# Linear attention and two gated layers on one core: batch 0 begun by pairs of heads, its spread over all rows, a late cast moved

## What is computed

```
kv  = k^T v                         per batch and head, 64 x 64
out = q kv;  out = out / sqrt(mean(out^2) + 1e-6) * g_norm
x   = out, heads side by side       4608 x 512
x   = (sigmoid(x Wg) * (x Wv)) Wo   512 -> 1536 -> 512
h   = x W_in                        512 -> 2048
y   = piecewise(h) W_out            h if h >= 1, 0 if h <= -1, else (h+1)^2/4;  2048 -> 512
```

## Time and profile before

| | |
|---|---|
| median of three runs | 1667.77 us |
| the profiled execution | 1663.86 us, of which its span 1662.1 us |
| busy in the span | PE 1645.1, DVE 1217.0, ACT 885.3, POOL 195.8 us |
| granted TensorE clock, mean | 1.00 |
| DMA | 278.91 MB, mean 168 GB/s |

### The profile page before, as it was taken

How to read it: one execution, slowest core, us unless ns; L and a number is a source line. 1 busy time by engine, 2 the same in 40 slices (tenths; PEclk the granted TensorE clock), 3 DMA queues, 4 the chain that set the end, 5 groups by cost and what they waited for, 6 DMA issues and landing times. The chain is left out here.

```text
span 1662.1 us, 31802 instructions
## 1 busy us (share of the span) xinstructions
PE 1645.1 (99%) x12471; PEld 1616.1 (97%) x12471; DVE 1217.0 (73%) x1733; ACT 885.3 (53%) x1612; POOL 195.8 (12%) x258
## 2 busy tenths in 40 slices
PE   8999999999999999999999999999999999999999
PEld 5899999999999999999999999999999999999999
DVE  5666777777877675876778887777777687766664
ACT  5666666655555554544445655555555444444442
POOL 2300001014432220100002400000001200000000
PEclk9999999999999999999999999999999999999999
DMA  7534444334776778745344433333438964444450
GB/s 269 179 125 144 132 148 142 114 130 133 253 250 232 245 241 288 248 157 155 117 143 140 165 129 143 118 118 136 167 143 267 341 185 135 129 128 127 128 137 29
DMA packets 229317, 278.91 MB, mean 168 GB/s; under 512 B 33072, under 2 KB 172848, under 8 KB 229168
## 3 DMA queue, kind: packets, MB, share of 16 engines
q1 hardware_dynamic: 217104, 233.35, 42.4%
q0 software_dynamic: 12064, 43.52, 8.2%
HBM read 156.76 MB, written 120.06 MB: 167 GB/s over the span
## 5 line engine op out<-in xcount | busy, mean ns | idle before, releaser
L1584 PE MATMUL x<-t_hi,v_lo 128*128 128x288 f32 x1664 | 495.8, 298 | 2.4 <-DVE v_lo L1104 0.9
L1585 PE MATMUL x<-t_lo,v_hi 128*128 128x288 f32 x1664 | 491.2, 295 | 0.0
L1586 PE MATMUL x<-t_hi,v_hi 128*128 128x288 f32 x1664 | 489.8, 294 | 0.0
L1584 PEld LDWEIGHTS x<-t_hi,v_lo 128*128 128x128 f32 x1664 | 312.0, 188 | 7.2 <-issue 2.1
L1586 PEld LDWEIGHTS x<-t_hi,v_hi 128*128 128x128 f32 x1664 | 313.3, 188 | 0.0
L1585 PEld LDWEIGHTS x<-t_lo,v_hi 128*128 128x128 f32 x1664 | 312.5, 188 | 0.1
L1584 PE MATMUL y<-t_hi,v_lo 128*128 128x288 f32 x832 | 248.2, 298 | 0.5 <-DVE c L1107 0.2
L1585 PE MATMUL y<-t_lo,v_hi 128*128 128x288 f32 x832 | 245.6, 295 | 0.0
L1586 PE MATMUL y<-t_hi,v_hi 128*128 128x288 f32 x832 | 245.0, 294 | 0.0
L1584 PE MATMUL x<-v_hi,t_lo 128*128 128x256 f32 x576 | 163.3, 283 | 2.7 <-ACT o_kept L1070 2.5
L1585 PE MATMUL x<-v_lo,t_hi 128*128 128x256 f32 x576 | 163.1, 283 | 0.0
(11 more groups left out here) (187 smaller groups left out, 3505.7 us busy)
## 6 DMA issues: line engine op xcount, KB each, us to landing
g_scratch<-c_tile SPq DMA_DIRECT2D x128, 288.0 KB, 2.4
gq<-g_scratch SPq DMA_DIRECT2D x64, 512.0 KB, 6.2
h_scratch<-gate SPq DMA_DIRECT2D x192, 144.0 KB, 2.0
hq<-h_scratch SPq DMA_DIRECT2D x32, 864.0 KB, 5.1
stage<-w_in POOLq DMA_DIRECT2D x68, 256.0 KB, 3.8
kv_ring<-kv_in SPq DMA_DIRECT2D x30, 512.0 KB, 4.4
fold_hi<-v_hi SPq DMA_DIRECT2D x14, 896.0 KB, 5.4
fold_lo<-v_lo SPq DMA_DIRECT2D x14, 896.0 KB, 6.9
```

The source lines that it names most:

```text
L1584: nc.tensor.matmul(dst, s_lo, m_hi, start=start, stop=False, skip_group_check=True)
L1585: nc.tensor.matmul(dst, s_hi, m_lo, start=False, stop=False, skip_group_check=True)
L1586: return nc.tensor.matmul(dst, s_hi, m_hi, start=False, stop=stop, skip_group_check=True)
```

## The change

Batch 0's k and v are loaded by pairs of heads, in 512-byte pieces, into places of their own; g's load is third. TensorE makes pair 0's and 1's products and heads, their two mean squares, then pairs 2 and 3, and the spread of the first two pairs before the second two pairs' means. A first root, reciprocal and inverse split serves pairs 0 and 1, a second all four. The warming passes behind the first ten are gone. The spread uses all 128 rows (the inverse's other rows are zeroed). The low part of task 0's weights and the sums of task 1's go from VectorE to GpSimd. Batch 1's k-v chunks have five places and no waits; its products are made in step 0; its k-v copies are ScalarE's. In stage D, the cast of item 4 comes after the first `keep`. The diff, cut:

```diff
         def _(sp):
-            def load_first_kv(i):
-                rows = min(P, S - i * P)
-                sp.dma_start(first_chunk(i)[0:rows, :], kv_in[0, i * P:i * P + rows, :]).then_inc(first_kv_loaded[i], 16)
+            def load_first_kv(c):
+                for side in range(2):
+                    at = slice(DM * side + P * c, DM * side + P * (c + 1))
+                    sp.dma_start(first_kv[:, 0:KVC - 1, at],
+                                 kv_in[0, 0:N, at].rearrange("(i p) d -> p i d", p=P)).then_inc(first_kv_loaded[c], 16)
...
-            for i in range(KVC):
-                load_first_kv(i)
-            for c in range(K):
-                load_query(first_query(c), 0, c, first_q_loaded[c])
-            sp.dma_start(g_col[:], g_in).then_inc(g_loaded, 16)
+            for c in range(K):
+                load_first_kv(c)
+                if c == 0:
+                    sp.dma_start(g_col[:], g_in).then_inc(g_loaded, 16)
+                    sp.dma_start(first_kv[0:REST, KVC - 1, :], kv_in[0, N:S, :]).then_inc(first_rest_loaded, 16)
+                load_query(first_query(c), 0, c, first_q_loaded[c])
+            for i in range(KVC):
+                load_kv(1, i)
...
         def _(pool):
+            make(nc.gpsimd.memset(inv_pair[:].bitcast(f32), 0.0))
+            def split_first():
+                pool.wait_ge(v_hi_done, 1)
+                for x in range(SEVEN):
+                    done = nc.gpsimd.tensor_tensor(v_lo[:, x, :], stage[:, 0, x, :], v_hi[:, x, :].bitcast(f32), ALU.subtract)
+                done.then_inc(v_ready, 1)
-            pool.wait_ge(first_kv_loaded[3], 16)
+            pool.wait_ge(first_kv_loaded[1], 32)
             load_task(0)
-            pool.wait_ge(first_q_loaded[1], 32)
+            pool.wait_ge(first_kv_loaded[3], 32)
             load_task(1)
...
-                if FOLD2_TASK <= task < C_TASK:
+                if task == 0:
+                    split_first()
+                elif FOLD2_TASK <= task < C_TASK:
                     sum_right(task)
-                elif task >= 2:
+                else:
                     sum_left(task)
...
         def _(act):
+            def copy_second_kv():
+                act.wait_ge(kv_used, KVC)
+                act.wait_ge(head_done, K)
+                for j in range(P // D):
+                    rows = slice(j * D, (j + 1) * D)
+                    nc.scalar.copy(kv_raw[rows, :, rows], M[rows, :].rearrange(
+                        "p (c e) -> p c e", c=K)[:, :, rows]).then_inc(kv_copied, 1)
...
-            square_heads(0, 0)
-            scale_heads(0, 0)
-            for c in range(1, K):
+            for c in range(2):
                 square_heads(0, c)
+                scale_heads(0, c)
+            root(0)
             split_weights(0)
-            scale_heads(0, 1)
-            root(0)
+            split_inverse(0)
+            square_heads(0, 2)
+            square_heads(0, 3)
+            split_item(0, 0)
+            root(1)
             scale_heads(0, 2)
             scale_heads(0, 3)
-            split_inverse(0)
+            split_item(0, 1)
+            split_inverse(1)
             split_weights(1)
-            split_item(0, 0)
-            split_item(0, 1)
...
-            for e in range(3, D_SLOTS):
-                split_d_item(e)
+            split_d_item(3)
...
+                if p == 0:
+                    split_d_item(4)
                 if p + D_SLOTS < len(SEQ):
...
         def _(dve):
+            def copy_first(c):
+                dve.wait_ge(first_kv_done, c + 1)
+                for j in range(P // D):
+                    rows = slice(j * D, (j + 1) * D)
+                    nc.vector.tensor_copy(kv_raw[rows, c, rows], first_bank(c)[rows, rows]).then_inc(kv_copied, 1)
...
-            copy_kv(0)
+            copy_first(0)
+            copy_first(1)
             sum_weights(0)
-            sum_weights(1)
-            split_weights(0)
+            copy_first(2)
             invert(0)
+            copy_first(3)
             split_inverse(0)
...
             sum_item(0, 1)
+            invert(1)
+            split_item(0, 1)
+            split_inverse(1)
             normalize_part(0, 2, 0)
             normalize_part(0, 3, 0)
-            split_item(0, 1)
...
-                if k == 0:
-                    copy_kv(1)
...
         def _(pe):
+            def first_pair(c):
+                pe.wait_ge(first_kv_loaded[c], 32)
+                if c == 2:
+                    pe.wait_ge(kv_copied, 2)
+                elif c == 3:
+                    pe.wait_ge(o_ready, 1)
+                for i in range(KVC):
+                    rows = min(P, S - i * P)
+                    if c == 0 and i == KVC - 1:
+                        pe.wait_ge(first_rest_loaded, 16)
+                    chunk = first_kv[:, i, :]
+                    last = nc.tensor.matmul(first_bank(c)[:, 0:P], chunk[0:rows, c * P:(c + 1) * P],
+                                            chunk[0:rows, DM + c * P:DM + (c + 1) * P],
+                                            start=i == 0, stop=i == KVC - 1, skip_group_check=True)
+                last.then_inc(first_kv_done, 1)
...
                     if (s, number) == (0, 1):
-                        kv_chunk(1, 3)
+                        kv_chunk(1, 0)
+                        kv_chunk(1, 1)
+                        pe.wait_ge(inv_ready, 2)
+                        pe.wait_ge(o_ready, K)
+                        pe.wait_ge(x_ready, 4)
+                        for c in (2, 3):
+                            for h in range(2):
+                                spread_part(0, c, h)
                     elif (s, number) == (0, 5):
-                        kv_chunk(1, 4)
+                        for i in range(2, KVC):
+                            kv_chunk(1, i)
...
             keep_warm(WARM_START)
-            for i in range(KVC):
-                kv_chunk(0, i)
-            keep_warm(WARM_COPY)
-            for c in range(K):
+            for c in range(2):
+                first_pair(c)
                 first_heads(0, c)
-            for c in range(K):
+            for c in range(2):
                 first_mean(0, c)
-            kv_chunk(1, 0)
-            kv_chunk(1, 1)
-            keep_warm(WARM_ROOT)
-            for c in range(K):
-                spread(0, c)
-                if c == 2:
-                    keep_warm(WARM_FIRST)
-            kv_chunk(1, 2)
+            for c in (2, 3):
+                first_pair(c)
+            for c in (2, 3):
+                first_heads(0, c)
+            pe.wait_ge(inv_ready, 1)
+            pe.wait_ge(spread_const, 1)
+            pe.wait_ge(o_ready, 2)
+            spread_part(0, 0, 0)
+            spread_part(0, 0, 1)
+            pe.wait_ge(kv_copied, 2 * K)
+            spread_part(0, 1, 0)
+            first_mean(0, 2)
+            pe.wait_ge(x_ready, 1)
+            spread_part(0, 1, 1)
+            first_mean(0, 3)
```

More of the change, by code:

```diff
@@ L17 @@
 EPS = 1e-6
[L18 removed]
+CONSTANTS = 8 + 2 * (P // D)
 PAIR = 32 + 2 * H
[L20 removed]
+WARM_START = 10
 C = S // 2
@@ L162, in program @@
         q_second = place("q_second", ATT2 + 4608, [P, 2, S])
+        first_kv = place("first_kv", V_HI + 14 * CHUNK * 4, [P, KVC, 2 * DM])
+        second_kv = place("second_kv", V_LO + 14 * CHUNK * 4, [P, KVC, 2 * DM])
+        first_q = [place(f"first_q{i}", at + 34 * CHUNK * 4, [P, 2, S]) for i, at in enumerate((V_HI, V_LO))]
         hq = [place(f"hq{x}", O + (6912 * x if x < 3 else 34688), [P, J1, C]) for x in range(4)]
@@ L194, in program @@
         warm_ready = sem("warm_ready")
-        first_kv_loaded = [sem(f"first_kv_loaded{i}") for i in range(KVC)]
+        first_rest_loaded = sem("first_rest_loaded")
+        first_kv_loaded = [sem(f"first_kv_loaded{c}") for c in range(K)]
+        first_kv_done = sem("first_kv_done")
+        second_kv_loaded = [sem(f"second_kv_loaded{i}") for i in range(KVC)]
         first_q_loaded = [sem(f"first_q_loaded{c}") for c in range(K)]
@@ L306, in head_banks, with first_bank, spread_bank @@
             return HB
+        def first_bank(c):
+            return (Z[0], Y[0], Z[0], HB[0])[c]
+        def spread_bank(n, c, h):
+            if n == 0:
+                return ((X[0], X[1]), (Z[0], X[0]), (HB[0], HB[1]), (X[1], Y[1]))[c][h]
+            return HB[h]
         def t_slot(r):
@@ L375, in load_kv @@
             def load_kv(n, i):
-                j = KVC * (n - 1) + i
-                sp.wait_ge(kv_used, j + 1 if j < 2 else j + 4)
                 rows = min(P, S - i * P)
-                sp.dma_start(kv_ring[0:rows, j % 2, :], kv_in[n, i * P:i * P + rows, :]).then_inc(kv_loaded[j % 2], 16)
+                src = kv_in[n, i * P:i * P + rows, :]
+                if n == 1:
+                    sp.dma_start(second_kv[0:rows, i, :], src).then_inc(second_kv_loaded[i], 16)
+                else:
+                    j = KVC * (n - 2) + i
+                    reach(sp, kv_used, KVC + j - 1 if j >= 2 else 0)
```

(22 more changed lines are left out.)

84 lines of the change are left out of this document (38 added, 46 removed).

## The result

| | before | after |
|---|---|---|
| median of 6 runs each, on one chip | 1668.28 us | 1656.61 us |
| lowest to highest | 1667.2 to 1670.47 | 1656.11 to 1656.96 |
| the profiled execution, its span | 1663.86, 1662.1 | 1656.11, 1654.3 |

The ratio is 0.9927 with a 95% interval of 0.9914 to 0.994: faster. The same kernel was run again beside others on two more chips: 1657.43 us against 1669.87 (0.9931, 0.9919 to 0.9944) and 1657.33 against 1666.65 (0.9938, 0.9924 to 0.9951). Three single executions of experiments 1 to 4 and of the kernel before beside them took 4.1, 5.6 and 9.1 ms in place of 1.67; they stand in no ratio and move no median by more than 0.3 us.

What follows compares the result with a forecast made beforehand. TensorE, busy 99% of the span, was taken as the bound. Gains of 0.95 us at the start and 0.1 at the late cast sum to 1.05, from the median 1667.77 to 1666.7 us; range 1662.9 to 1669.8.

Steps and rivals of the forecast that it cites:

- At nothing: List of edits priced at no time, among them the spread over 128 rows, wider constants and removed warming passes.
- The premise behind it: Whole kernel: TensorE is busy 99% of the span, so only the 17 us in which it idles can yield gain.
- The start: Up to step k = 1 of the first MoE stage: its first product at 37.3 instead of 38.27, 0.95 us earlier.
- The landing: Start: weight task 0, asked for by GpSimd at 8.4, lands 7.2 us later; 15.2 taken, range 12.9 to 15.6.
- The charge for the port: Start: GpSimd and VectorE meeting at SBUF cost 0.4 us each, before and behind product one; bounds 0 and 2 us.
- The late cast: Change to the last stage: the 2.46 us stall goes, VectorE's chain takes most back; gain 0.1, bounds 0 and 0.25.
- The median: Whole kernel: the forecast gain was taken off the median of three timed runs, 1667.77, 3.9 above the profiled execution.
- rival 4: Start: without warming passes TensorE's clock falls from 2.4 to 1.2 GHz, costing 6 us more, 1672.8; chance 0.05.
- Rival 1: Start: small pieces load like large ones, weights land at 12.9, no port meetings; 3.85 us earlier, 1663.9; chance 0.27.

Runs made afterwards that it cites:

- experiments 1: Kernel before with only the spread's ones and inverse covering all 128 rows, rows 48 and up zero; 1658.31 us, ratio 0.9956.
- experiment 2: Kernel after with the spread back on 48 rows, all else as changed; 1666.42 us, ratio 1.0005.
- Experiment 3: Kernel before with only the cast of item 4 moved behind the first keep; 1665.12 us, ratio 0.9989.
- experiment 4: Kernel after with item 4's cast back ahead of the loop; 1659.51 us, ratio 0.996, all five runs at mean clock 0.997 or 0.998.
- 7: Kernel after with the spread over 80 rows instead of 128; 1658.53 us, ratio 0.9943 against the kernel before.
- 8: Kernel after with the spread over 64 rows instead of 128; 1665.55 us, ratio 0.9995 against the kernel before.
- experiment 6: Kernel before with the spread over 128 rows and item 4's cast moved, nothing of the new start; 1658.11 us, ratio 0.9939.
- 5: Kernel after, unchanged, run again beside others on another chip; 1657.43 us.

## Why the prediction was wrong

**The step that failed** stands under "At nothing": "The spread over 128 rows instead of 48 streams the same 288 columns." It does, and that is worth nothing only if the time of a matmul among others is its columns. The runs show 0.38 us for each pair of 64 rows or fewer between ones of 80 or more, 22 pairs and 8.2 us in all, eight times the gain that I forecast. The premise behind it failed too: "any gain has to come from the 17 us of the span in which it is not" busy. These 8.2 us lay in the 99% in which it is. Experiments 1 and 2 put them on the spread and nothing else, 7 and 8 on the border in rows. It stood in the trace of before: 0.22 instead of 0.13, and a weight load with idle time and no releaser. I had read PE's waits and left out this place since PE counts as busy there.

The Trainium skill (TensorEngine Tiling (Array Packing), Key Properties) says that changing the tiling mode drains the engine. It doesn't say there that a matmul of 64 rows or fewer is such a change, and no trace names a mode. If it is one, the runs agree, and the way from 128 rows to 64 and back is 0.38 us here. By that rule the edit had a gain where I priced none.

**Columns** are less simple. The mean squares' weights are 48 columns wide on 128 rows. From batch 2 on they are float32r, and their four matmuls follow the products and each other 0.13 us apart, at no cost. Batch 1's are plain float32, and the trace of before shows there what it shows at the 48-row spread:

```profile
39.04 0.29 PE L1586 MATMUL x<-t_hi,v_hi 128*128 128x288 f32 x1
39.26 1.17 PE L1637 MATMUL m<-sq,head_cols 128*48 128x288 f32 x4
40.36 0.40 PE L1584 MATMUL y<-t_hi,v_lo 128*128 128x288 f32 x1
40.60 0.30 PE L1585 MATMUL y<-t_lo,v_hi 128*128 128x288 f32 x1
...
41.14 0.29 PE L1586 MATMUL y<-t_hi,v_hi 128*128 128x288 f32 x1
41.27 1.13 PE L1630 MATMUL h<-q_ring,kv_raw 128*128 128x288 f32 x4
42.02 0.51 PE L1584 MATMUL x<-t_hi,v_lo 128*128 128x288 f32 x1
42.37 0.29 PE L1585 MATMUL x<-t_lo,v_hi 128*128 128x288 f32 x1
```

The four records of 48 columns start 0.22 behind their neighbour and take 1.56 us from first to last line, the four of 128 columns beside them 0.13 and 1.23: 0.33 more. The kernel after has the same 1.56 in this place, so it is no part of this change, and no experiment was made on it.

**The start** was right by its own steps in the profiled execution: weights land 15.4 (forecast 15.2), product one 24.53 (24.2), first product of k = 1 37.58 (37.3), 0.69 earlier (0.95). The landing was right by luck: GpSimd asked at 9.29 instead of 8.4 and had the weights 6.1 us later instead of 7.2. GpSimd's seven subtractions took 5.07 us. The charge for the port (0.8) was about right: beside GpSimd, VectorE's low parts took 0.56, 0.96 and 0.86 us instead of 0.45, 0.76 and 0.45, 0.7 more together. But one execution was too little. In the other two profiles of the kernel after, that product starts at 38.60 and 39.10. The kernel before has 38.27, and with the spread and the late cast 38.42. So the moment scatters by 1.5 us, more than the gain, and experiments 2 and 6 show no gain of the start that could be told from none.

**The late cast** was forecast at 0.1 within 0 and 0.25. The mechanism was as described: the old wait goes, others come in its place. Its bounds were too narrow: over all profiles the waits at this place add up to between 1.9 and 3.9 us with the old order (three profiles) and 1.8 and 3.2 with the new one. That they hang on when the quarter lands is likely, but not shown.

**The median.** I added the 3.9 us between the profiled execution of before and its median to the forecast. The six runs of the kernel after lie within 0.9 us of each other, at clock 1.000. The 3.9 is most likely a lower granted clock in part of the start, though no trace and no clock of those three runs is on record. Experiment 3's profile, 6 us above the one of before, shows what it looks like (by stretch; the clock is the third number from the end):

```profile
5.00:10.00 5.00, 3.38 (x26) 2.96 (x24) 0.00 (x0) 2.53 (x3) 1.22 (x2) 1.00 1.03 311
10.00:15.00 5.00, 4.51 (x20) 3.13 (x21) 0.84 (x2) 0.00 (x0) 2.29 (x4) 0.69 1.07 391
15.00:20.00 5.00, 5.00 (x14) 3.65 (x13) 2.10 (x6) 2.20 (x6) 0.00 (x0) 0.63 0.72 266
20.00:25.00 5.00, 5.00 (x21) 2.46 (x19) 2.40 (x4) 3.79 (x7) 0.00 (x0) 1.00 0.21 60
```

At 0.69 and 0.63 the level is 1.2 GHz instead of 2.4 for 6.8 of these ten microseconds (11.9 to 18.7). PE is busy 0.68 of the 5 us ahead of them, then 0.90 and 1.00. From 31 us on this execution is 3.7 us behind the one of before. This was rival 4's fear, but it comes with the old start too. Of 45 runs of the kernel before on the three chips of the experiments 8 have a mean clock of 1.000, of the kernel after's 16 in all 12. But with the old start, experiment 3 has it in 6 of 9 runs and experiment 6 in 4 of 6, and with the new one experiment 2 in 3 of 9 and experiment 4 in none of 5. So neither start nor cast sorts the kernels, and why the kernel before shows the lower clock more often is open. I had no experiment on it. Between the median spans of the runs at 1.000 the gain is 7.2 us (1661.4 to 1664.5 against 1654.3 to 1656.4), so of the 11.7 between the medians of the first table the other 4.5 us are put down to the clock by argument and not by a trace; over the three pairs with a ratio the medians differ by 9.3 to 12.4.

**The rivals.** None of the five named the spread. Rival 1 had a time (1663.9) nearest to the measured one for a wrong reason.

## What to carry to other kernels

Look where the number of rows of consecutive matmuls crosses the border between 64 and 80: each excursion cost about 0.4 us here, for two matmuls of 288 columns as for four of 128, so fill the operand with zeros to 128 rows, or put the short ones side by side (the 48-row pair with the 64-row chunk behind it paid once). Look at plain float32 matmuls with narrow weights too. Compare the starts of neighbouring matmuls with the usual distance, as "busy" hides such a gap. Price an edit that "streams the same" against the trace all the same, and take a start that hangs on DMA landings from several executions before crediting it with less than 2 us.

## What the runs showed of the hardware that I had not expected

- Summing over 48 or 64 rows between 128-row matmuls costs 0.38 us per excursion, over 80 rows nothing (0.91 or 0.92 against 0.53 from the product ahead to the second behind); four matmuls of 64 rows in a row pay once. Weights of 48 columns on 128 rows cost nothing in float32r and 0.33 us in plain float32.
- A load of 116 rows of 4 KB is far slower than one of 112 or 128: the fifth load of batch 1, behind four of 116 rows, landed 28.6 us after its issue, where the 64-row one of the kernel after took 11.7 and a 112-row one behind rows of 128 and 112 took 15.1. The stretch from 17 to 22 us moved 109 GB/s in place of 386, and the whole kernel took 67 us more. Why it is that number was not taken apart.
- The granted clock fell to 0.50, the level of 1.2 GHz, in some executions of most of the kernels: at 11.9 to 18.7 us in one profile, at 20.8 to 24.2, 34.3 to 37.7 and 30.6 to 34.0 in three others, with TensorE busy 1.00 of these stretches. In four profiles (experiments 1, 3, 4 and 5) it fell within 1.3 us behind a wait of 1.9 to 3.9 us at the change to stage D; in the profile of before, which has one of 2.46 there, it did not.
